# Partial sums of two units on GpSimd, one shift on GpSimd, and other orders ahead of the first matrix product of a fused attention and expert kernel

## The reference

```python
scores = np.where(masks, scale * q @ k.T, -1e9)
scores = scores - np.max(scores, axis=-1, keepdims=True)
attn = np.exp(scores)
attn = attn / (np.sum(attn, axis=-1, keepdims=True) + 1e-09)
x = attn @ v                       # rearranged to 2304 x 512
h = x @ w_in                       # 512 -> 2048
g = np.where(h >= 1, h, np.where(h <= -1, 0.0, (h + 1) ** 2 / 4.0))
x = g @ w_out                      # 2048 -> 512
skip_score = x @ w_skip            # rows with a score over 0 go through one of 8 experts
```

## Time and profile before

| | us |
|---|---|
| median of 3 runs | 509.23 (508.8 to 510.26) |
| the profiled execution | 509.0 |
| its span | 507.1 |
| TensorE busy | 494.7 |
| VectorE, ScalarE, GpSimd busy | 254.0, 194.3, 212.7 |
| prologue, until `hidden(0)` starts | 29.5 |

### The profile page before, as it was taken

One profiled execution on the slowest core, in us unless ns is written; L12 is line 12 of the kernel. 1 busy time (PEld: TensorE's weight loads), 2 busy tenths in 40 slices (PEclk: granted clock), 3 DMA queues, 4 the chain that ended last, 5 costly groups with the idle time before them and its releaser, 6 DMA issues.

```text
span 507.1 us, 8897 instructions
## 1 busy us (share of the span) xinstructions
PE 494.7 (98%) x3423; PEld 427.8 (84%) x3427; DVE 254.0 (50%) x595; ACT 194.3 (38%) x435; POOL 212.7 (42%) x235
## 2 busy tenths in 40 slices
PE   8899999999999999999999999999999999999994
PEld 4588888889989888888888888888998898888993
DVE  5976656733335636676525667652434333223222
ACT  4975655543223324343423343442322223222222
POOL 0669876662223224465423555642223222131320
PEclk9899999999999999999999999999999999999998
DMA  8992211103001204202110420000300026740001
GB/s 274 344 388 113 73 39 43 52 2 124 1 1 48 74 25 172 78 4 79 50 48 17 156 80 34 1 2 17 125 0 1 1 87 260 278 166 1 2 1 65
DMA packets 18977, 42.15 MB, mean 83 GB/s; under 512 B 2054, under 2 KB 3920, under 8 KB 18932
## 3 DMA queue, kind: packets, MB, share of 16 engines
q1 hardware_dynamic: 18580, 41.13, 23.7%
q10 hardware_dynamic: 256, 0.41, 0.2%
q0 software_dynamic: 96, 0.02, 0.0%
HBM read 32.94 MB, written 8.78 MB: 82 GB/s over the span
## 4 chain that ended last, share of the span: by engine, by line
PE 90%; DVE 4%; ACT 3%; issue 1%; DMA 1%; POOL 1%; DVEq 0%
PE bank L1046 39%; PE bank L1030 39%; PE bank L832 4%; PE bank L869 3%; PE bank L849 3%; ACT prob_first L1560 1%; DMA qk<-in_qk_dram 1%; PE bank L973 1%; PE bank L954 1%; POOL prob_first L1725 1%; DVE prob L1181 1%; DVE prob_first L1165 0%; DVE sum_terms L1191 0%; DVE row_max L1169 0%; ACT g_hi L1687 0%
## 5 line engine op out<-in xcount | busy, mean ns | idle before, releaser
L1790 POOL TENSOR_TENSOR g_lo<-act_f,g_hi 128x384 fp32r<-128x384 f32 x96 | 97.4, 1015 | 196.7 <-ACT g_hi L1687 196.2
L1678 ACT ACTIVATE act_f<-act_f,half_col 128x384 f32<-128x384 f32 x96 | 59.1, 616 | 200.8 <-DVE act_f L1417 200.8
L1417 DVE TENSOR_SCALAR act_f<-bank 128x384 f32<-128x384 f32 x96 | 53.4, 556 | 146.4 <-PE bank L1030 141.5
L1030 PE MATMUL bank<-x_hi,win_hi 128*128 128x384 f32 x384 | 87.7, 347 | 0.6 <-DVE act_f L1420 0.6
L1046 PE MATMUL bank<-wout_hi,g_hi 128*128 128x512 f32 x285 | 85.0, 406 | 0.0
L1687 ACT CAST g_hi<-act_f 128x384 fp32r<-128x384 f32 x96 | 49.1, 512 | 92.1 <-DVE act_f L1420 91.9
L1030 PE MATMUL bank<-x_hi,win_lo 128*128 128x384 f32 x384 | 83.9, 337 | 0.0
L1030 PE MATMUL bank<-x_lo,win_hi 128*128 128x384 f32 x384 | 83.1, 334 | 0.0
L1046 PE MATMUL bank<-wout_lo,g_hi 128*128 128x512 f32 x285 | 81.1, 393 | 0.0
L1046 PE MATMUL bank<-wout_hi,g_lo 128*128 128x512 f32 x285 | 81.0, 392 | 0.0
L1030 PEld LDWEIGHTS bank<-x_hi,win_hi 128*128 128x128 f32 x384 | 66.7, 188 | 8.3 <-issue 1.5
(11 more groups left out here) (130 smaller groups left out, 423.4 us busy)
## 6 DMA issues: line engine op xcount, KB each, us to landing
w_early<-in_w_dram SPq DMA_DIRECT2D x4, 2048.0 KB, 8.7
qk<-in_qk_dram SPq DMA_DIRECT2D x12, 592.0 KB, 5.1
out_dram<-y_rows SPq DMA_DIRECT2D x18, 256.0 KB, 2.6
win_raw<-in_w_in_dram SPq DMA_DIRECT2D x16, 256.0 KB, 9.4
wout_raw<-in_w_out_dram SPq DMA_DIRECT2D x16, 256.0 KB, 9.6
y_dram<-y_rows SPq DMA_DIRECT2D x15, 256.0 KB, 3.2
v<-in_v_dram SPq DMA_DIRECT2D x6, 384.0 KB
v<-in_v_dram SPq DMA_DIRECT2D x6, 288.0 KB
```

The source lines that it names most:

```text
L1030: mm = pe.matmul(h_ps[s % 2][:, 0:CH], w[:, f, P * k:P * (k + 1)], x[:, k, cols], start=(at == 0), stop=(at == len(order) - 1))
L1417: dve.tensor_scalar(tile, h_ps[s % 2][:, 0:CH], -1.0, 1.0, ALU.max, ALU.min).then_inc(clip_ready, 1)
L1678: act.activation(tile, tile, ACT.Square, bias=half_col[:, 0:1], scale=0.5).then_inc(square_ready, 1)
L1790: pool.tensor_tensor(g_lo[:, s % RING, :], act_f[:, s % 2, :], g_hi[:, s % RING, :].bitcast(F32), ALU.subtract).then_inc(g_lo_ready, 1)
```

## The change

- GpSimd gets two new jobs ahead of its scalings: K0 and K1 (`sum_probs`). For each head of units 0 and 1 it adds the right half of each block's 128 columns to the left half, and then the right half of that 64 to the left one, into a new buffer `part_sums`. VectorE's E0 and E1 then reduce the remaining 32 columns of both heads in one instruction. `sums_done` gives the new counts of `sum_steps`.
- The last prologue unit (5) is shifted by GpSimd (D5, `shift_scores`), and ScalarE takes its exponentials in two instructions instead of eight. A new semaphore, `first_shift_ready`, carries this.
- The four orders change: VectorE does M2 ahead of E0, M3 ahead of E1 and so on, and all E ahead of L0; ScalarE does X2 and X3 ahead of C0, and W0 behind X4; TensorE does V3 ahead of P4.
- The fillers change from 34 to 28: none ahead of P1 and P4, eight ahead of P0, two ahead of V1, one each ahead of P2, P3 and P5.
- VectorE's wait for `row_skips` in `keep_sums` goes, and so does VectorE's branch hint; TensorE keeps its own.

```diff
-PE_BEFORE = "S0 S1 S2 S3 S4 P0 S5 P1 V0 P2 V1 P3 V2 P4 V3 P5 V4 V5"
-DVE_BEFORE = "M0 M1 E0 M2 E1 M3 M4 E2 E3 M5 E4 L0 E5 L1 L2 L3 L4 L5"
-ACT_BEFORE = "X0 X1 X2 C0 X3 C1 X4 C2 H0 X5 C3 H1 W0 H2 C4 H3 C5 H4 H5 W1 W2"
-POOL_BEFORE = "G0 G1 G2 G3 G4 G5 R0 R1 R2"
-FILLERS = {("P", 0): 4, ("S", 1): 4, ("S", 2): 9, ("P", 1): 4, ("P", 2): 5, ("P", 3): 2, ("P", 4): 2, ("P", 5): 2, ("V", 4): 2}
+PE_BEFORE = "S0 S1 S2 S3 S4 P0 S5 P1 V0 P2 V1 P3 V2 V3 P4 P5 V4 V5"
+DVE_BEFORE = "M0 M1 M2 E0 M3 E1 M4 E2 M5 E3 E4 E5 L0 L1 L2 L3 L4 L5"
+ACT_BEFORE = "X0 X1 X2 X3 C0 X4 W0 C1 C2 H0 X5 C3 H1 H2 H3 C4 C5 H4 H5 W1 W2"
+POOL_BEFORE = "K0 K1 G0 G1 G2 D5 G3 G4 G5 R0 R1 R2"
+FILLERS = {("S", 1): 4, ("S", 2): 9, ("P", 0): 8, ("P", 2): 1, ("V", 1): 2, ("P", 3): 1, ("P", 5): 1, ("V", 4): 2}
...
+        def sums_done(n):
+
+            return 3 * (n + 1) if n < POOL_SUMS else 4 * (n + 1) - POOL_SUMS
...
             def reciprocal_sums(n):
                 u = UNITS[n]
+                if n < POOL_SUMS:
+                    dve.wait_ge(part_sums_ready, 2 * n + 2)
+                    dve.tensor_reduce(sum_terms[0:unit_rows(u), :, 0:u.nt, 0], part_sums[:, n, :, :, 0:TK // 4],
+                                      AX.X, ALU.add).then_inc(sum_steps, 1)
...
-                        dve.wait_ge(row_skips, CT * c)
...
-                if s == HINT_STEP:
-                    the_end_is_likely = dve.mark_branch_hint_location()
...
-            for_tiles(dve, first, tile, the_end_is_likely)
+            for_tiles(dve, first, tile)
...
-                    if n < N_PRO:
+                    if SHIFTED <= n < N_PRO:
+                        act.wait_ge(first_shift_ready, 2 * (n - SHIFTED) + hh + 1)
+                        a = act.activation(prob_of(u, hh), prob_of(u, hh), ACT.Exp)
+                    elif n < SHIFTED:
...
+            def sum_probs(n):
+
+                u = UNITS[n]
+                half, quarter = TK // 2, TK // 4
+                for hh in range(2):
+                    parts = part_sums[:, n, hh, :, :]
+                    pool.wait_ge(exp_ready, 2 * n + hh + 1)
+                    pool.tensor_tensor(parts, tiled(u, hh)[:, :, 0:half], tiled(u, hh)[:, :, half:TK], ALU.add)\
+                        .then_inc(half_sums, 1)
+                    pool.wait_ge(half_sums, 2 * n + hh + 1)
+                    pool.tensor_tensor(parts[:, :, 0:quarter], parts[:, :, 0:quarter], parts[:, :, quarter:half],
+                                       ALU.add).then_inc(part_sums_ready, 1)
```

More of the change, by code:

```diff
@@ L89 @@
 N_PRO = 6
+SHIFTED = 5
+POOL_SUMS = 2
 REST = 2
@@ L323, in build @@
         at += 2 * 512
+        part_sums = sb("part_sums", [TQ, POOL_SUMS, 2, 4, TK // 2], F32, offset=at)
+        at += POOL_SUMS * 4 * 2 * 4 * TK // 2
         assert at <= steps_end
@@ L454, in build @@
         masked_ready = sem("masked_ready")
+        first_shift_ready = sem("first_shift_ready")
         shift_ready = sem("shift_ready")
@@ L457, in build @@
         sum_steps = sem("sum_steps")
+        half_sums, part_sums_ready = sem("half_sums"), sem("part_sums_ready")
         prob_ready = sem("prob_ready")
@@ L1188, in reciprocal_sums @@
                 u = UNITS[n]
[L1189 to L1192, removed]
+                if n < POOL_SUMS:
+                    dve.wait_ge(part_sums_ready, 2 * n + 2)
+                    dve.tensor_reduce(sum_terms[0:unit_rows(u), :, 0:u.nt, 0], part_sums[:, n, :, :, 0:TK // 4],
+                                      AX.X, ALU.add).then_inc(sum_steps, 1)
+                else:
+                    for hh in range(2):
+                        dve.wait_ge(exp_ready, 2 * n + hh + 1)
+                        dve.tensor_reduce(sum_terms[0:unit_rows(u), hh, 0:u.nt, 0], tiled(u, hh), AX.X, ALU.add)\
+                           .then_inc(sum_steps, 1)
+                dve.wait_ge(sum_steps, sums_done(n) - 2)
                 sums = row_sum[0:unit_rows(u), u.n % 8, :, 0:u.nt]
-                dve.wait_ge(sum_steps, 4 * n + 2)
                 dve.tensor_reduce(sums, sum_terms[0:unit_rows(u), :, 0:u.nt, :], AX.X, ALU.add).then_inc(sum_steps, 1)
-                dve.wait_ge(sum_steps, 4 * n + 3)
+                dve.wait_ge(sum_steps, sums_done(n) - 1)
                 dve.reciprocal(sums, sums).then_inc(sum_steps, 1)
@@ L1718, in shift_scores @@
                     pool.tensor_tensor(tiled(u, hh), tiled(u, hh), over_tiles(u, peak_of(u, hh)), ALU.add)\
-                        .then_inc(shift_ready, 1)
+                        .then_inc(first_shift_ready if n < N_PRO else shift_ready, 1)
+            def sum_probs(n):
+                u = UNITS[n]
+                half, quarter = TK // 2, TK // 4
+                for hh in range(2):
+                    parts = part_sums[:, n, hh, :, :]
[5 more added lines that the diff above has]
+                                       ALU.add).then_inc(part_sums_ready, 1)
             def scale_probs(n):
@@ L1723, in scale_probs @@
                 for hh in range(2):
-                    pool.wait_ge(sum_steps, 4 * n + 4)
+                    pool.wait_ge(sum_steps, sums_done(n))
                     pool.tensor_tensor(tiled(u, hh), tiled(u, hh), over_tiles(u, sums_of(u, hh)), ALU.mult)\
@@ L1777, in _ @@
             for kind, n in jobs_of(POOL_BEFORE):
+                if kind == "K":
+                    sum_probs(n)
+                if kind == "D":
+                    shift_scores(n)
                 if kind == "G":
```

## The result

The changed kernel takes 505.77 us (median of 10 runs, 503.76 to 508.22), the kernel before 509.06 (10 runs, 508.52 to 510.26). The ratio is 0.9931, with a 95% interval of 0.991 to 0.9952. The forecast was 508.3 us and a range from 507.2: the kernel is faster than its lower end.

The account below looks back on a forecast made before the run. TensorE's work was taken as the bound, counted from the start of `hidden(0)`, with GpSimd deciding until unit 1's transposes. That start moves from 29.49 to 28.55 us, the tail adds zero: 509.23 - 0.94 = 508.3 us, range 507.2 to 509.9.

Parts of the forecast that it names:

- Below zero I see no reason beyond 0.1 us: Tail: removing VectorE's hint at the last branch was taken as zero effect, with at most 0.1 us to save.
- costs nothing today: Loop: the removed row_skips wait was said to cost nothing, as VectorE itself has already waited for those semaphore steps.
- GpSimd's adds: Prologue, partial sums of units 0 and 1: 0.74 us per 256-element add and 0.47 per 128-element add.
- G0: Prologue, GpSimd's scaling of unit 0: queued behind the new sums, it would start at 14.95 us instead of 13.12.
- P0 at 16.05: Prologue: TensorE's transposes of unit 0 would start at 16.05 us, where they ran at 14.21 before.
- The fillers as TensorE's own time: Prologue: fillers cost TensorE 0.23 us each, so six fewer between the first values product and `hidden(0)` save 1.4 us.
- Rival A: Prologue: GpSimd's adds are dearer than worked out, delaying everything until unit 1's transposes; 508.7 to 509.4 us, chance 0.14.
- rival B: Prologue: TensorE's clock stays low for longer after its idle time; 509.5 us, or 510.6 if it lasts further; chance 0.08.
- rival D: Prologue: more gain, as the clock doesn't fall and adds are cheap; 507.8 us, 507.3 without TensorE's last holes; chance 0.17.
- The forecast's own case: Prologue: low clock as in the profiled execution, with a gain of 0.4 to 1.4 us; chance 0.57.
- a second hold-up between P0 and V1: Prologue: TensorE held up again between unit 0's transposes and unit 1's values product would decide for rival B.
- The sum of 0.94 us: Prologue: `hidden(0)` would start at 28.55 us instead of 29.49, and the whole gain would be kept to the end.

Follow-up runs that it names:

- the second profile: Profile of the changed kernel run once more with nothing altered; that run measured 506.2 us (8 runs).
- the run with 14 fillers: The changed kernel with 14 fillers in place of 8 ahead of the first transposes (P0): 504.14 us, ratio to the kernel before 0.991.
- the runs at an equal tail: The old kernel without its five row_skips waits (median 506.1 us) against the changed kernel (506.1 us); also both with long tails, 508.8 to 509.1 against 508.26.

## Why the prediction was wrong

**The step that failed is the tail.** "Below zero I see no reason beyond 0.1 us": a saving of 2.5 us lay there. I had read 5.07 us behind VectorE's last instruction and asked only whether an engine with the hint could become as slow as the others without it. I took the other engines' branches as the measure of the tail without having a row that showed who ended it. It was VectorE, 3.6 us behind its branch. The rule of the Trainium skill that I cited points at the right place and I applied it to one side only: I asked what a missing hint could cost, not whether a stall was being paid already. And the removed wait, "costs nothing today", is right for where it stood; its worth was in the instructions it took up: without the waits the old program has 1012 instructions in place of 1016. With the rest of the change it has 1009, below the edge.

**What of the prologue was right.** GpSimd's adds: 0.74 and 0.47 us forecast, 0.726 and 0.453 measured. The remaining reduce: 0.41, measured 0.406. Two whole exponentials instead of eight, 0.44 each: 0.458. D5: 0.76 at most, measured 1.28 us for both. G0 came behind the adds, at 14.81 us in the second profile for 14.95 forecast. That this fits so well is in part luck: the first add started at 8.89 and not at 9.8, and GpSimd then stood idle for 1.02 us between K0 and K1, where I had the four halves in one piece. P0 at 16.05: 15.90 in the second profile, where the 16 products of S0 and of S1 took 1.12 us each, and 17.39 in the first, where they took 2.02. The fillers as TensorE's own time: 1.4 to 1.7 us measured for the 1.5 worked out. Rival A (dear adds) is out.

**What of it was off.** The forecast had one value for the low clock, 3.4 us under P1 and V0 as before, and 12.5 us from P0 to `hidden(0)`. The profiles have 11.81 with no low clock, 13.05 with 3.4 us of it and 14.21 with 6.8: rival B and rival D, which I had given 0.08 and 0.17, each hold in some executions of the same kernel. The forecast's own case (3.4 us) is 0.55 us dearer than worked out. There the low clock lies under P1, V0 and P2 and no longer under P1's fillers, and V0's products take 76% more time at it (1.55 for 0.88 us), not some 40%. The point from which B was to decide, a second hold-up between P0 and V1, is open: the second profile has one, 0.34 us ahead of P2, but the clock had fallen 3.7 us earlier, behind the waits around P0. The sum of 0.94 us was not kept in the median, where 0 to 0.8 us are left. That it is lost to the low clock is supported by the spans by mean clock above, and by the run with 14 fillers, which changes nothing but the idle time ahead of P0: 504.14 us. It is a median of six on one chip, and the changed kernel's own best times (503.7) are as low, as they should be if the fillers only make them common.

**How the total comes about.** 509.06 - 505.77 = 3.3 us: 2.5 of tail, and the rest, 0.8, is the prologue's part and what remains of chance between sets of runs. That the rest lies near the forecast gain of 0.94 is no confirmation of it, as the runs at an equal tail differ by 0 to 0.8.

## What to carry to other kernels

When a stretch at the end has no busy engine, find out who ends it before calling anything there free: if it is an engine that comes late out of a taken branch, the length of that engine's program, dead code included, can be worth more than an edit of its work. A pipeline that is freed from its slow engine begins to hang on TensorE's clock, so fill the wait ahead of the part that now decides, up to the moment at which its operands come. And compare several profiles of the same kernel before putting one number on a prologue whose clock and transfers vary.

## What the runs showed of the hardware

- Behind a taken branch VectorE needed 0.6 us to its next instruction with a program of up to 1012 instructions, and 3.6 to 3.9 us with 1015 to 1017. Eight instructions that are never executed cost 2.1 us in the median. The branch hint made no difference to the tail on either side of the edge.
- The same first product groups took different times in different executions of one kernel: S1's 16 products took 2.02 us in one profile of the changed kernel and 1.12 in the other. The granted clock reads 1.00 in both, so the cause stays open. In the faster one S1's operands came late:

```profile
7.97 1.12 PE L844 MATMUL bank<-qk 64*96 64x128 f32 x16 [1.52 <-DMA qk<-in_qk_dram]
```

- At a granted clock of 0.50, the level of 1.2 GHz, the 16 products of V0 take 1.55 us, and at 1.00 0.88.
- After the waits around P0 (0.3 to 2.6 us ahead of it, 0.4 to 0.5 between its halves) the clock fell to 0.50 for 3.4 or 6.8 us in seven profiles. It didn't fall in the first profile of the changed kernel, and did in the second.
